# A transformer block in fp32: the first MLP product by a seven-product scheme over two batches, activations kept transposed, attention in pairs of heads

## Chip, cores, metric

The kernel runs on one core of a Trainium2 chip. The metric is the device time of one launch in microseconds (us), as the median over runs. A profile is one execution of the program, recorded by the hardware profiler.

## The reference

Inputs are q, k, v of 4 batches, 12 heads, 448 positions and 64 columns a head, and two MLPs of width 768 with 3072 hidden units. Everything is fp32.

```python
# attention, per batch and head
q_n, k_n = rmsnorm(q, g_q), rmsnorm(k, g_k)
attn = softmax(q_n @ k_n.T / sqrt(64))
x = attn @ v                                  # heads side by side: 4 x 448 x 768
# first MLP, behind a layer norm
xn = (x - mean(x)) / sqrt(var(x) + 1e-6) * g_ln
x = x + maximum(xn @ w_ch1, 0) @ w_ch2        # 768 -> 3072 -> 768
# second MLP, behind a mixing of positions of rank 32
u = x + (x.T @ U @ V).T
out = u + maximum(u @ w_ch1b, 0) @ w_ch2b
```

## The kernel before

**Number format.** A large product is made of three matmuls in the single-pass format float32r: an operand is split into a high part (a copy by ScalarE, written as float32r) and a low part (a subtraction by VectorE), and high x high, high x low and low x high are added up in PSUM. Transposes and the product of the softmax weights with v are plain fp32.

**Attention** (function `attention`, L105 to L557) runs over 48 heads, a loop of steps with software pipelining: each engine has its own `step`, in which it works on up to four heads at different stages. The order on TensorE is written out by hand in `step` (L337): scores of head n-1 (L296, L297), transposes of the exponentials of head n-2 (L308), products with v of heads n-3 and n-2 (L322), transposes of K of head n (L333). For the scores the high and low part of q lie one above the other, 128 rows, and K is held twice (L274), so that a tile of scores needs two matmuls of 448 columns, against the high and the low part of K. ScalarE computes the exponentials (L372), VectorE the maxima (L444), copies half of the transposed weights out of PSUM (L463) and makes low parts (L469, L476). POOL squares q and K (L249), takes the root of the means with a power (L253, L267) and normalises K (L271). SP issues all loads. The result x stays in SBUF in natural layout, positions on partitions.

**MLPs** (function `mlps`, L560 to L956) are 8 stages, one for each MLP and batch. A stage loops over 24 tiles j of 128 hidden units: `hidden` (L721) makes one hidden tile in 18 matmuls of 448 columns (6 tiles of the input x 3 terms, L733), ScalarE and VectorE apply the maximum with zero and split it (L817, L932), and `output` (L737) adds its part to the six PSUM banks of the output in 18 more (L750). The hidden tile of j+1 comes ahead of the output of j, so that TensorE need not wait. Weights of one j (two transfers of 384 KB, L98 and L99) are loaded once for each batch and split anew each time: two high parts of 768 columns on ScalarE (L781, L782), two low parts on VectorE (L844, L845). They wait for ring slots (`w_free`). Between output tiles TensorE does side work (`side`, L684): it transposes the finished output of the stage before back to natural layout (L680), where VectorE adds it to x (L891), mixes positions (L698, L706) and, at the end of a stage, transposes the next batch's input (L669), which ScalarE and VectorE split (L786, L851, L854). The first batch's input is built after the attention (L658). At the end the last output is transposed back (L680), added (L891) and stored (L832).

## Time and profile before

| | |
|---|---|
| runs, device time | 1797.34, 1797.57, 1797.84 us; median 1797.57 |
| profiled execution, span from its first to its last instruction | 1794.6 us |
| TensorE busy | 1766.4 us, 98% |
| VectorE, ScalarE, POOL busy | 913.4, 706.3, 202.1 us |
| read from and written to memory | 173.5 MB, 5.5 MB |
| first matmul of an MLP product | 344.8 us |
| granted TensorE clock, mean | 0.998 |

The page of the profiled execution gives its span alone. The median of the runs is 2.97 us above it: what lies around the span. A matmul's recorded duration holds its way through the pipeline, so the distance between starts tells what one costs. In a row, L750 is line 750 of the kernel, PE is TensorE, DVE VectorE, ACT ScalarE.

### The profile page before, as it was taken

The page shows a single profiled execution, that of the slowest core. Times are in us where ns is not written, and L with a number is a line of the kernel's source. Part 1 is how long each engine was busy: PE and PEld are TensorE (multiplying, and loading weights), DVE is VectorE, ACT ScalarE, POOL GpSimd, SP SyncE. Part 2 cuts the span into 40 slices and gives each one's busy share as a digit, 9 for nine tenths or more (in the row PEclk, how much of TensorE's full clock was granted, in tenths as well). Part 3 has the DMA queues.
Part 4 walks back from the last instruction along what each step waited for, and adds up shares of the span by engine and source line. Part 5 has one row for each costly group of instructions (what it writes and reads, how often), then busy time and mean ns, then how long its engine had stood idle before and what let it go on. Part 6 is the DMA issues. An engine that isn't in the chain of part 4 may idle for free.

```text
span 1794.6 us, 29017 instructions
## 1 busy us (share of the span) xinstructions
PE 1766.4 (98%) x10272; PEld 1655.9 (92%) x10272; DVE 913.4 (51%) x1595; ACT 706.3 (39%) x1268; POOL 202.1 (11%) x201
## 2 busy tenths in 40 slices
PE   6999999999999999999999999999999999999998
PEld 5999999899999999999999999999999999999997
DVE  7999999743344444444444444444433433343332
ACT  5777777522333323332333233323222322232221
POOL 6666666000000000000000000000000000000000
PEclk9999999999999999999999999999999999999999
DMA  2222224233333233333333333332433333333320
GB/s 73 69 69 72 68 71 139 87 106 116 113 106 103 93 111 101 106 106 106 105 108 100 102 100 106 106 106 89 138 121 106 97 131 121 106 99 128 121 88 31
DMA packets 205744, 180.41 MB, mean 101 GB/s; under 512 B 12497, under 2 KB 179281, under 8 KB 205649
## 3 DMA queue, kind: packets, MB, share of 16 engines
q1 hardware_dynamic: 203280, 173.51, 30.3%
q10 hardware_dynamic: 2368, 5.51, 0.8%
q8 instruction: 75, 1.23, 0.3%
q14 instruction: 21, 0.16, 0.0%
HBM read 173.48 MB, written 5.51 MB: 100 GB/s over the span
## 4 chain that ended last, share of the span: by engine, by line
PE 80%; DVE 0%; issue 0%; ACT 0%
PE h_ps L733 39%; PE y_ps L750 38%; PE h_ps L680 1%; PE h_ps L669 1%; PE h_ps L698 1%; PE h_ps L706 0%; PE y_ps L658 0%; DVE in_nat L891 0%; ACT in_hi L786 0%; DVE in_lo L854 0%; DVE in_lo L851 0%; DVE y_t L927 0%
## 5 line engine op out<-in xcount | busy, mean ns | idle before, releaser
L844 DVE TENSOR_TENSOR w_lo<-w_raw,w_hi 128x768 fp32r<-128x768 f32 x190 | 182.0, 958 | 674.0 <-ACT w_hi L782 674.0
L750 PE MATMUL y_ps<-h_hi,w_hi 128*128 128x448 f32 x1152 | 424.4, 368 | 0.0
L733 PE MATMUL h_ps<-in_hi,w_hi 128*128 128x448 f32 x1152 | 415.9, 361 | 3.1 <-DVE in_lo L851 1.1
L733 PE MATMUL h_ps<-in_hi,w_lo 128*128 128x448 f32 x1152 | 417.9, 363 | 0.0
L750 PE MATMUL y_ps<-h_hi,w_lo 128*128 128x448 f32 x1152 | 417.8, 363 | 0.0
L750 PE MATMUL y_ps<-h_lo,w_hi 128*128 128x448 f32 x1152 | 417.7, 363 | 0.0
L733 PE MATMUL h_ps<-in_lo,w_hi 128*128 128x448 f32 x1152 | 417.4, 362 | 0.0
L781 ACT ACTIVATE w_hi<-w_raw 128x768 fp32r<-128x768 f32 x189 | 159.7, 845 | 538.1 <-PE y_ps L750 538.1
L817 ACT ACTIVATE h_hi<-h_ps 128x448 fp32r<-128x448 f32 x192 | 104.7, 545 | 380.1 <-PE h_ps L733 338.5
L733 PEld LDWEIGHTS h_ps<-in_hi,w_hi 128*128 128x128 f32 x1152 | 215.6, 187 | 19.1 <-DVE in_lo L851 1.5
L733 PEld LDWEIGHTS h_ps<-in_lo,w_hi 128*128 128x128 f32 x1152 | 216.2, 188 | 15.8
L750 PEld LDWEIGHTS y_ps<-h_lo,w_hi 128*128 128x128 f32 x1152 | 216.7, 188 | 14.0
L750 PEld LDWEIGHTS y_ps<-h_hi,w_hi 128*128 128x128 f32 x1152 | 215.9, 187 | 13.5
L750 PEld LDWEIGHTS y_ps<-h_hi,w_lo 128*128 128x128 f32 x1152 | 216.1, 188 | 13.0
L733 PEld LDWEIGHTS h_ps<-in_hi,w_lo 128*128 128x128 f32 x1152 | 216.1, 188 | 12.4
L845 DVE TENSOR_TENSOR w_lo<-w_raw,w_hi 128x768 fp32r<-128x768 f32 x190 | 180.7, 951 | 0.0
L322 PEld LDWEIGHTS av_ps<-v_nat,e_t 112*112 112x112 f32 x1536 | 172.7, 178 | 5.2
L322 PE MATMUL av_ps<-v_nat,e_t 112*112 112x64 f32 x1536 | 174.2, 257 | 0.0
L782 ACT ACTIVATE w_hi<-w_raw 128x768 fp32r<-128x768 f32 x189 | 156.4, 827 | 0.0
L932 DVE SCALAR_TENSOR_TENSOR h_lo<-h_ps,h_hi 128x448 fp32r<-128x448 f32 x192 | 118.9, 619 | 71.6 <-ACT h_hi L817 70.9
L372 ACT ACTIVATE e_nat<-scores,nbias,rs_all 112x448 f32<-112x448 f32 x192 | 138.0, 721 | 40.3 <-DVE nbias L452 40.2
L444 DVE TENSOR_REDUCE nmax<-scores 112x1 f32<-112x448 f32 x192 | 113.2, 615 | 4.3 <-PE scores L297 1.6
(90 smaller groups left out, 1407.3 us busy)
## 6 DMA issues: line engine op xcount, KB each, us to landing
w_raw<-in_moe_w_ch SPq DMA_DIRECT2D x384, 384.0 KB, 3.8
qk_raw<-in_q SPq DMA_DIRECT2D x48, 112.0 KB, 2.0
qk_raw<-in_k SPq DMA_DIRECT2D x48, 112.0 KB, 2.1
qt_raw<-in_q_t SPq DMA_DIRECT2D x48, 112.0 KB, 2.5
v_nat<-in_v SPq DMA_DIRECT2D x48, 112.0 KB, 2.0
out<-o_nat ACTq DMA_DIRECT2D x12, 336.0 KB, 5.0
out<-in_nat ACTq DMA_DIRECT2D x4, 336.0 KB, 3.1
u_sb<-in_moe_U SPq DMA_DIRECT2D x4, 56.0 KB, 2.5
```

The lines of the kernel that those rows point to most:

```text
L322: last = nc.tensor.matmul(av_ps[:TP, m * D:(m + 1) * D], e_t[:, m, c, :], v_nat[:, slot, c, :], start=(c == 0), stop=(c == NI - 1))
L372: nc.scalar.activation(e_nat[:, i, :], scores[i][:TP, :S], ACT.Exp, bias=nbias[:, i:i + 1], scale=rs_all[:, ds(g, 1), i:i + 1].rearrange(" ...
L444: nc.vector.reduce_max(nmax[:, i:i + 1], scores[i][:TP, :S], axis=AX, negate=True).then_inc(rawmax_done, 1)
L669: last = nc.tensor.transpose(h_ps[c % 2][:, i * TP:(i + 1) * TP], in_nat[:, i, c * P:(c + 1) * P], ident[:TP, :TP])
L733: last = nc.tensor.matmul(h_ps[j % 2][:, :S], w[:, j % NW, c, :], x[:, c, :], start=(c == 0 and t == 0), stop=(c == DC - 1 and t == 2))
L750: last = nc.tensor.matmul(y_ps[c][:, :S], w[:, j % NW, c * P:(c + 1) * P], x[:, j % 2, :], start=(j == 0 and t == 0), stop=(j == FC - 1 an ...
L781: nc.scalar.activation(w1_hi[:, r], w1_raw[:, r], ACT.Copy)
L782: nc.scalar.activation(w2_hi[:, r], w2_raw[:, r], ACT.Copy).then_inc(w_hi_done, 1)
L817: nc.scalar.activation(h_hi[:, j % 2, :], h_ps[j % 2][:, :S], ACT.Relu).then_inc(hhi_done, 1)
L844: nc.vector.tensor_tensor(w1_lo[:, r], w1_raw[:, r], w1_hi[:, r].bitcast(F32), ALU.subtract)
L845: nc.vector.tensor_tensor(w2_lo[:, r], w2_raw[:, r], w2_hi[:, r].bitcast(F32), ALU.subtract).then_inc(w_lo_done, 1)
L932: nc.vector.scalar_tensor_tensor(h_lo[:, j % 2, :], h_ps[j % 2][:, :S], 0.0, h_hi[:, j % 2, :].bitcast(F32), ALU.max, ALU.subtract).then_i ...
```

## The change

The kernel is rewritten. The parts on which the steps of the prediction rest:

- **Products.** A stage now holds one MLP and two batches: 4 stages. The two batches, the two halves of the 768 inputs and two hidden tiles make a 2 x 2 x 2 block product, done by Strassen's scheme in the form with 7 products (named P1 to P7) of sums of blocks instead of 8. Each is 3 input tiles x 3 terms, 9 matmuls of 448 columns. There are 12 groups a stage. POOL makes 4 sums of weight blocks a group (`weight_sum`, 384 columns), ScalarE and VectorE split 7. P2, P3 and P4 accumulate onto the banks of P1, P5 and P7. VectorE combines the rest with 5 adds (`combine`), ScalarE copies P1 out (`keep_p1`), and 4 hidden tiles get their high and low parts. The second product stays plain: after each 2 groups 12 products of 12 matmuls, of which each second closes two banks that VectorE adds to the residual (`gather`). Splits are done 3 to 4 products ahead of use, in a ring of 8. A weight transfer is now one of 786 KB for 7 or for 6 products (a run), requested two products before the end of the run before the last, into one of two buffers.
- **Inputs of a stage.** They are sums of blocks too: for each of 3 tiles 4 sums on POOL (`make_sums`), 7 high parts on ScalarE and 7 low parts on VectorE (448 columns), made during the last second product of the stage before, and for the first stage in steps 66 to 97 of the attention (of 96 steps and 6 of draining). Normalised x and x go through memory (`xnrm`, `xres`), 229 KB a tile.
- **Transposed activations.** x is transposed once after the attention and once more normalised (4 transposes a pair each, for the last 6 pairs normalised during the first stage). Outputs are never transposed back; the host lays the result out. The residual of a stage (`acc`, 2.75 MB) is loaded from memory from the 8th product of a stage on (`load_acc`). The mixing is done in stages 1 and 2 in 12 items that last 22 products each: 8 transposes, 8 matmuls of 256 columns, 2 of 448.
- **Attention in pairs of heads.** 24 pairs x 4 steps. For the scores the two heads lie in rows 0 to 63 and 64 to 127; a step has 3 terms x 2 heads of 64 rows, alternating between the heads, into two banks. One maximum on VectorE reads both banks (896 columns), the root on POOL has 16 columns, K of both heads is transposed together (4 transposes a pair). The low part of q is made by POOL. TensorE runs the scores of step n, then values of step n-2 and transposes of step n-1 for either head.
- **Idle TensorE fed.** Matmuls whose result is not used (`warm`): 36 before the first transposes, 5 after them, 13 in steps 1 to 3. The first products of the first stage are placed between the last steps of the attention (`seq`).

The diff, cut to these parts:

```diff
+P1, P7, P6, P5, P2, P3, P4 = range(7)
+ORDER = (P1, P7, P6, P5, P2, P3, P4)
+ONTO = {P2: P1, P3: P5, P4: P7}
+LAST_IN_BANK = (P6, P2, P3, P4)
+
+OUTS = ((0, 0), (1, 0), (2, 0), (0, 1), (1, 1), (2, 1), (3, 0), (3, 1), (4, 0), (4, 1), (5, 0), (5, 1))
...
+    prods = []
+    for s in range(STAGES):
+        for j in range(NJ):
+            for g in (2 * j, 2 * j + 1):
+                prods += [("G", s, g, k) for k in ORDER]
+            prods += [("M", s, j, n) for n in range(len(OUTS))]
...
+    make_at = {}
+    for c, first in enumerate((66, 77, 88)):
+        for off in range(-2, 8):
+            make_at.setdefault(("step", first + off + off // 3), []).append((0, c, off))
+    for s in range(1, STAGES):
+        first = number["M", s - 1, NJ - 1, 0]
+        for c in range(HC):
+            for off in range(-2, 8):
+                make_at.setdefault(("prod", first + (0, 3, 5)[c] + off), []).append((s, c, off))
...
+    seq = []
+    for n in range(STEPS):
+        seq.append(("step", n))
+        if 58 <= n < 63:
+            seq.append(("pre", n - 63))
+        if n >= N:
+            seq.append(("prod", n - N))
+    seq += [("prod", q) for q in range(STEPS - N, Q)]
...
+                def load_weights(r):
+                    if r >= len(runs):
                         return
+                    if r >= 2:
+                        sp.wait_ge(wlo_done, runs[r - 2][-1] + 1)
+                    kind, s, n, k = prods[runs[r][0]]
+                    src = w1[s // 2, n].rearrange("p a c -> p (a c)") if kind == "G" else w2[s // 2, n, k // 6]
+                    sp.dma_start(w_raw[r % 2][:].rearrange("p a c -> p (a c)"), src).then_inc(w_in[r % 2], 16)
...
+                def load_acc(s):
...
+                    for b in range(2):
+                        sp.dma_start(acc[:, b], xres[2 * (s % 2) + b].rearrange("c p s -> p c s")).then_inc(acc_in, 16)
...
+                def root(t):
+                    pool.wait_ge(ms_done, t + 1)
...
+                    nc.gpsimd.tensor_tensor(rs[:, t % 2].rearrange("p a h i -> p (a h i)"), qk_ms[:],
+                                            m_half[:TP], ALU.pow).then_inc(rs_done, 1)
...
+                def norm_k(t):
+                    pool.wait_ge(rs_done, t + 1)
+                    nc.gpsimd.tensor_tensor(kn.rearrange("p i (h d) -> p h i d", h=2), qk[:, t % 2, 1],
+                                            rs[:, t % 2, 1].unsqueeze(3).to_broadcast([TP, 2, NI, D]),
+                                            ALU.mult).then_inc(kn_done, 1)
...
+                def weight_sum(r, k):
+                    weights_in(pool, r)
...
+                    if k == P5:
+                        if old is not None:
+                            pool.wait_ge(wlo_done, product_of(old, P5) + 1)
+                        out, in0, in1, op = w_s1[:], a21, a22, ALU.add
+                    if k == P7:
+                        pool.wait_ge(sum_done, sum_no[r, P5] + 1)
+                        out, in0, in1, op = a21, a11, a21, ALU.subtract
+                    if k == P6:
+                        if old is not None:
+                            pool.wait_ge(wlo_done, product_of(old, P3) + 1)
+                        pool.wait_ge(sum_done, sum_no[r, P5] + 1)
+                        out, in0, in1, op = w_s2[:], w_s1[:], a11, ALU.subtract
+                    if k == P3:
+                        pool.wait_ge(sum_done, sum_no[r, P6] + 1)
+                        pool.wait_ge(wlo_done, product_of(r, P6) + 1)
+                        out, in0, in1, op = w_s2[:], a12, w_s2[:], ALU.subtract
+                    nc.gpsimd.tensor_tensor(out, in0, in1, op).then_inc(sum_done, 1)
...
+                def score(n):
+                    t, i = divmod(n, NI)
                     if i == 0:
-                        pe.wait_ge(klo_done, g + 1)
-                        pe.wait_ge(qlo_done, g + 1)
-                    wait(pe, exp_done, NI * g + i - NI + 1)
-                    lhs = q_st[:, slot, i * TP:(i + 1) * TP]
-                    nc.tensor.matmul(scores[i][:TP, :S], lhs, k_hi[:, slot, :], start=True, stop=False)
-                    nc.tensor.matmul(scores[i][:TP, :S], lhs, k_lo[:, slot, :], start=False,
-                                     stop=True).then_inc(scores_done, 1)
-
-                def turn_exp(pair, n, m):
-
-                    if not real(pair, n):
-                        return
-                    g = head(pair, n)
-                    pe.wait_ge(exp_done, NI * g + m + 1)
-                    wait(pe, et_odd if m % 2 else et_even, 2 * g + m // 2)
+                        emptied(pe, "k", t)
+                        pe.wait_ge(qlo_done, t + 1)
+                    wait(pe, exp_done, 2 * (n - 1))
+                    for a, b in ((q_hi, k_hi), (q_hi, k_lo), (q_lo, k_hi)):
+                        for h in range(2):
+                            rows = slice(h * D, (h + 1) * D)
+                            last = nc.tensor.matmul(mm_ps[:TP, 2 * (n % 2) + h, :S], a[rows, t % 2, i * TP:(i + 1) * TP],
+                                                    b[rows, t % 2], start=a is q_hi and b is k_hi, stop=a is q_lo)
+                    last.then_inc(s_done, 1)
+
...
+                def value(n, h):
...
+                    emptied(pe, "e", n, h)
+                    cols = slice((h * NI + i) * D, (h * NI + i + 1) * D)
                     for c in range(NI):
+                        last = nc.tensor.matmul(mm_ps[:TP, 4 + t % 2, cols], e_t[h][:, c * TP:(c + 1) * TP],
+                                                v[:, t % 2, h, c], start=c == 0, stop=c == NI - 1)
+                    last.then_inc(val_done, 1)
...
+                def product(q):
+                    kind, s, n, k = prods[q]
...
+                            read_out(pe, *old)
+                    w = w_hi[:, q % RING], w_lo[:, q % RING]
+                    if kind == "G":
+                        for c in range(HC):
+                            if n == 0:
+                                pe.wait_ge(inlo_done[c], made(s, k))
+                            for p, (a, x) in enumerate(((0, in_hi), (0, in_lo), (1, in_hi))):
+                                last = nc.tensor.matmul(bank(q), w[a][:, c * P:(c + 1) * P], x[:, k, c],
+                                                        start=k not in ONTO and c == 0 and p == 0,
+                                                        stop=c == HC - 1 and p == 2, skip_group_check=k in ONTO)
+                    else:
+                        d, half = OUTS[k]
+                        if d == 0:
+                            pe.wait_ge(hlo_done, 4 * (s * NG + 2 * n + half + 1))
+                        for b in range(2):
+                            for c in range(2):
+                                for p, (a, x) in enumerate(((0, h_hi), (0, h_lo), (1, h_hi))):
+                                    last = nc.tensor.matmul(bank(q, b), w[a][:, c * P:(c + 1) * P], x[:, half, 2 * c + b],
+                                                            start=half == 0 and c == 0 and p == 0,
+                                                            stop=half == 1 and c == 1 and p == 2)
+                    last.then_inc(prod_done, 1)
...
+                def mixing(item, off):
+                    i, part = divmod(off - 7, 3)
...
+                        pe.wait_ge(xslo_done, NI * item + i + 1)
+                        for x in (xs_hi, xs_lo):
+                            last = nc.tensor.matmul(sc_ps[1][:, :2 * P], u_st[:, i].rearrange("p n r -> p (n r)"), x[:],
+                                                    start=i == 0 and x is xs_hi, stop=i == NI - 1 and x is xs_lo)
+                        last.then_inc(z_done, 1)
...
+                            wait(pe, mu_done, 2 * item)
+                        wait(pe, xslo_done, NI * item + i)
+                        for e in range(2):
+                            last = nc.tensor.transpose(sc_ps[0][:TP, e * P:(e + 1) * P], xa[:, e, i * TP:(i + 1) * TP],
...
+                            pe.wait_ge(v_ok, 1)
+                        pe.wait_ge(mixlo_done, item + 1)
+                        for e in range(2):
+                            nc.tensor.matmul(sc_ps[e][:, :S], mix[:, e * P:(e + 1) * P], v_mx[:], start=True,
+                                             stop=True).then_inc(mo_done, 1)
...
+                def warm(times):
+                    for _ in range(times):
+                        nc.tensor.matmul(mm_ps[:, 5, :P], ident[:], ident[:], start=True, stop=True)
...
+                warm(36)
+                turn_k(0)
+                warm(5)
+                for what, n in seq:
+                    if what == "step":
+                        if n < N:
+                            score(n)
+                        if 1 <= n <= 3:
+                            warm((7, 3, 3)[n - 1])
+                        for h in range(2):
+                            if 0 <= n - 2 < N:
+                                value(n - 2, h)
+                            if 0 <= n - 1 < N:
+                                turn_e(n - 1, h)
+                        if n % NI == 2 and n // NI + 1 < NP_:
+                            turn_k(n // NI + 1)
+                        if xt_pair(n) is not None:
+                            turn_x("x", xt_pair(n))
+                        if xn_pair(n) is not None:
+                            turn_x("n", xn_pair(n))
+                    if what == "prod":
+                        if ln3_pair(n - 2) is not None:
+                            turn_x("n", ln3_pair(n - 2))
+                        if (at := mix_of(n)):
+                            mixing(*at)
+                        product(n)
...
+                def maximum(n):
+                    t, i = divmod(n, NI)
...
+                    nc.vector.reduce_max(nmax[:, n % 2], mm_ps[:TP, 2 * (n % 2):2 * (n % 2) + 2, :S], axis=AX,
+                                         negate=True).then_inc(max_done, 1)
...
+                    nc.vector.tensor_tensor(nbias[:, n % 2], nmax[:, n % 2], rs[:, t % 2, 0, :, i],
+                                            ALU.mult).then_inc(nb_done, 1)
...
+                def weight_low(q):
+                    dve.wait_ge(whi_done, q + 1)
+                    w = width(q)
+                    nc.vector.tensor_tensor(w_lo[:, q % RING, :w], weights(q), w_hi[:, q % RING, :w].bitcast(F32),
+                                            ALU.subtract).then_inc(wlo_done, 1)
...
+                def combine(q):
+                    g, k = g_no(q), prods[q][3]
+                    if k not in COMB or k == P7:
+                        return
+                    dve.wait_ge(prod_done, q + 1)
+                    if k == P6:
+                        dve.wait_ge(p1_done, g + 1)
+                        nc.vector.tensor_tensor(t_u2, bank(q), t_u2, ALU.add).then_inc(comb_done, 1)
+                        dve.wait_ge(comb_done, 5 * g + 1)
+                        wait(dve, hlo_done, 4 * g)
+                        nc.vector.tensor_tensor(t_c22, bank(number[prods[q][:3] + (P7,)]), t_u2, ALU.add
+                                                ).then_inc(comb_done, 1)
+                        return
+                    if k == P5:
+                        dve.wait_ge(comb_done, 5 * g + 2)
+                        nc.vector.tensor_tensor(t_c22, bank(q), t_c22, ALU.add).then_inc(comb_done, 1)
+                    if k == P3:
+                        nc.vector.tensor_tensor(t_c12, bank(q), t_u2, ALU.add).then_inc(comb_done, 1)
+                    if k == P4:
+                        nc.vector.tensor_tensor(t_c21, bank(q), t_u2, ALU.add).then_inc(comb_done, 1)
...
+                def gather(q):
+                    _, s, j, k = prods[q]
+                    d, half = OUTS[k]
+                    if not half:
+                        return
+                    dve.wait_ge(prod_done, q + 1)
+                    if s and j == 0 and d == 0:
+                        dve.wait_ge(acc_in, 32 * s)
+                    for b in range(2):
+                        nc.vector.tensor_tensor(acc[:, b, d], bank(q, b), acc[:, b, d], ALU.add).then_inc(ev_done, 1)
```

## Rows read from the trace of the kernel before

**Rows 1.** The page, busy time of each engine in us, its share, instructions.

```profile
PE 1766.4 (98%) x10272; PEld 1655.9 (92%) x10272; DVE 913.4 (51%) x1595; ACT 706.3 (39%) x1268; POOL 202.1 (11%) x201
```

**Rows 2.** Two stretches: busy us and instructions by engine, granted clock, DMA share, GB/s.

```profile
100.00:200.00 100.00, 100.00 (x915) 95.99 (x913) 94.75 (x229) 78.05 (x184) 63.50 (x63) 1.00 0.25 70
...
500.00:1000.00 500.00, 498.85 (x2568) 466.60 (x2567) 223.52 (x329) 166.12 (x255) 2.01 (x2) 1.00 0.32 103
```

**Rows 3.** The page, lines of the chain that ended last, share of the span.

```profile
PE h_ps L733 39%; PE y_ps L750 38%; PE h_ps L680 1%; PE h_ps L669 1%; PE h_ps L698 1%; PE h_ps L706 0%; PE y_ps L658 0%; DVE in_nat L891 0%; ACT in_hi L786 0%; DVE in_lo L854 0%; DVE in_lo L851 0%; DVE y_t L927 0%
```

**Rows 4.** Groups of TensorE instructions: shapes, count, busy us, mean ns, idle before.

```profile
L733 PE MATMUL h_ps<-in_lo,w_hi 128*128 128x448 f32 x1152 | 417.4, 362 | 0.0
...
L322 PE MATMUL av_ps<-v_nat,e_t 112*112 112x64 f32 x1536 | 174.2, 257 | 0.0
...
L308 PE MATMUL et_ps<-ident,e_nat 112*112 112x112 f32 x768 | 98.5, 261 | 0.4 <-ACT e_nat L372 0.4
```

**Rows 5.** Timeline of one head in attention, TensorE: start us, us.

```profile
199.72 0.44 PE L296 MATMUL scores<-k_hi,q_st 128*112 128x448 f32 x1
...
200.20 0.55 PE L308 MATMUL et_ps<-ident,e_nat 112*112 112x112 f32 x4
...
200.59 0.91 PE L322 MATMUL av_ps<-v_nat,e_t 112*112 112x64 f32 x8
...
201.34 0.56 PE L333 MATMUL kt_ps<-ident,kn 112*128 112x112 f32 x4
...
201.66 0.44 PE L296 MATMUL scores<-k_hi,q_st 128*112 128x448 f32 x1
...
201.94 0.36 PE L297 MATMUL scores<-k_lo,q_st 128*112 128x448 f32 x1
...
206.30 0.44 PE L296 MATMUL scores<-k_hi,q_st 128*112 128x448 f32 x1
```

**Rows 6.** Pieces of the chain in order of time: start us, us.

```profile
344.79 7.22 PE h_ps L733 x36
...
534.84 3.61 PE y_ps L750 x18
542.38 3.61 PE y_ps L750 x18
...
1777.60 7.22 PE y_ps L750 x36
```

**Rows 7.** Groups of VectorE and ScalarE instructions, columns as in Rows 4.

```profile
L372 ACT ACTIVATE e_nat<-scores,nbias,rs_all 112x448 f32<-112x448 f32 x192 | 138.0, 721 | 40.3 <-DVE nbias L452 40.2
L932 DVE SCALAR_TENSOR_TENSOR h_lo<-h_ps,h_hi 128x448 fp32r<-128x448 f32 x192 | 118.9, 619 | 71.6 <-ACT h_hi L817 70.9
L444 DVE TENSOR_REDUCE nmax<-scores 112x1 f32<-112x448 f32 x192 | 113.2, 615 | 4.3 <-PE scores L297 1.6
...
L900 DVE TENSOR_TENSOR xs_lo<-x_all,xs_hi 112x384 fp32r<-112x384 f32 x32 | 16.9, 549 | 0.0
```

**Rows 8.** POOL: two groups of instructions, columns as in Rows 4.

```profile
L249 POOL TENSOR_TENSOR qk_sq<-qk_raw 112x512 f32<-112x512 f32 x47 | 48.9, 1040 | 0.0
...
L649 POOL TENSOR_TENSOR rstd<-var_eps,m_half 112x4 f32<-112x4 f32 x3 | 3.0, 1007 | 468.1 <-DVE var_eps L868 468.1
```

**Rows 9.** Timeline of the start, POOL and VectorE, and TensorE's first score.

```profile
9.28 1.64 POOL L267 TENSOR_TENSOR rs_all<-qk_ms,m_half 112x8 f32<-112x8 f32 x1 [1.50 <-DVE qk_ms L488]
...
14.14 0.62 DVE L476 TENSOR_TENSOR q_st<-qt_raw,q_st 64x448 fp32r<-64x448 f32 x1
14.19 2.07 POOL L267 TENSOR_TENSOR rs_all<-qk_ms,m_half 112x8 f32<-112x8 f32 x1 [1.00 <-DVE qk_ms L488]
...
15.53 0.71 PE L296 MATMUL scores<-k_hi,q_st 128*112 128x448 f32 x1 [6.00 <-DVE k_lo L469]
```

**Rows 10.** Timeline of the end: the last adds on VectorE.

```profile
1789.74 1.02 DVE L891 TENSOR_TENSOR in_nat<-h_ps,x_all 112x384 f32<-112x384 f32 x2 [0.17 <-PE h_ps L680]
```

**Rows 11.** The page, DMA issues: out<-in, queue, count, KB each, us to landing.

```profile
w_raw<-in_moe_w_ch SPq DMA_DIRECT2D x384, 384.0 KB, 3.8
```


## Prediction before the result

> **What bounds the kernel now.** I read the page's busy line first, then stretches, then the chain, then single instructions. TensorE is busy for 98% of the span [rows 1]; attention and MLP stretches separately show it at 100% and 99.8%, with VectorE at 95% in attention but 45% in the MLPs, and the granted clock at 1.00 in both [rows 2], which is the upper of its two levels, 2.4 GHz. The chain of waits has 77% of the span in the two product lines L733 and L750 [rows 3]. Busy time is modelled, so I take the pace from starts. Eighteen matmuls of a product take 3.61 us and 36 take 7.22 us [rows 6], so one costs 0.200 us although its row says 362 ns [rows 4]. In attention one head lasts from 199.72 to 206.30, 6.58 us [rows 5]. Inside it nothing is missing: 4 transposes take 0.39 us (0.098 each), 8 value matmuls 0.75 (0.094 each), the 4 of K 0.32 (0.08 each) [rows 5]. The value line has 1536 matmuls for 48 heads [rows 4], so each of the 16 of a head is two instructions. 32 values are 3.0 us, 16 transposes 1.6, K 0.3, which leaves 1.7 for 8 scores, 0.21 each. TensorE bounds everything, and the time is a count of its instructions.
>
> By stage: first product matmul at 344.8 [rows 6]; then 6912 of them x 0.200 = 1382; the last 36 start at 1777.60 and end at 1784.8, so the MLP stretch of 1440 us holds 58 us of other work. One piece of it: two neighbouring blocks lie 7.54 us apart where 36 matmuls need 7.20 [rows 6], so three transposes cost 0.34. After 1784.8 come 9.8 us of tail, the last two adds starting at 1789.74 [rows 10].
>
> **The products.** One group is two hidden tiles for two batches. It cost 2 x 2 x 18 = 72 matmuls and costs 7 products x 9 = 63. 4 stages x 12 groups x 63 = 3024 against 3456. The second product stays at 4 x 6 x 12 x 12 = 3456. 6480 x 0.200 = 1296, 86 us less. This is the main gain.
>
> What must hide behind it. VectorE, per group: 5 combining adds and 4 low parts at 0.62 (448 columns, L932), 7 weight splits of 384 columns at 0.55 (L900) [rows 7]: 9.4 us of the 12.6 that TensorE needs. ScalarE has 12 copies; at 0.72, what an exponential of 448 columns costs [rows 7], they are 8.6, an upper bound. POOL: 4 sums of 384 columns; 512 columns take 1.04 [rows 8], so about 0.8 each, 3.3 in all. The tightest wait is P3, which accumulates onto P5's bank: P5 ends 1.8 us before P3 begins, and VectorE has a 0.55 split (done while P5 still runs) and the 0.62 add in between, so 1.0 us is left. All is covered: cost nothing. If that slack goes, each group pays the excess. The second product has 28.8 us per j for 12 splits of 256 columns (0.15 + 256 x 1.04 ns = 0.42, by the line through L900 and L444 [rows 7]) and 12 adds of 0.62: 12.5.
>
> **Other TensorE work in the MLPs.** Gone: the transposes back and those that build inputs. Added: 12 mixing items of 8 transposes (0.113 each with switching, from the 0.34), 8 matmuls of 256 columns (0.13; between 0.094 and 0.200), 2 of 448, 7 interruptions of 0.07: 2.8 us each, 34; 6 late transpositions, 3. Together 37, before 58.
>
> **Stalls at the seams.** Inputs of the next stage are made during the last second product: 21 VectorE subtractions of 0.62 = 13.0 beside its own 12.5, so 25.5 of 28.8. POOL adds 12 sums at 0.93 = 11. What both engines do to each other is in the trace. The root over 8 columns takes POOL 1.64 us at 9.28, and 2.07 us at 14.19, where VectorE began a two-operand subtraction at 14.14 [rows 9]: it lost 0.43 us to an instruction of 0.62. If all of it excluded each other a seam would need 36.7 us of 28.8, 7.9 late; if none, 0. I take 4 for each of 3 seams. The Trainium skill, SBUF — State Buffer, section Who interferes with whom, calls this an exclusive lock of the port that the two engines share; the trace agrees with those 0.43 us. The reload of the 2.75 MB residual starts 12.6 us into a stage and is wanted at about 35; 384 KB land in 3.8 us [rows 11], so even seven one after another take 27, and one behind the other on the queue about 13. Between 0 and 5 us a stage I take 2. Seams and reloads: 18.
>
> **Attention.** Per pair of heads, TensorE now: 64 values 6.0; 32 + 4 + 3 transposes (weights, x, normalised x in 18 of 24 pairs) x 0.098 = 3.8; K 0.3, since both heads share 128 columns; and 24 score matmuls of 64 rows. No row of the trace has two matmuls in the array at once. Bounds: two heads together, 12 x 0.21 + 4 x 0.08 for a fresh start = 2.8; one after another, 24 x 0.21 + 0.3 = 5.3. The nearest rows, matmuls of full height, come one after another, but those compete for the same rows of the array; these two use different halves and write different banks, so I take 2.8 and keep 5.3 as a rival. Pair: 12.9. VectorE per pair: 4 maxima of 896 columns (1.08, by the same line) with their bias 0.2, 4 copies 0.61, the sum of squares 1.4, the output 0.7, statistics 1.1, K 0.7, small 0.6: 12.0. It must follow TensorE step by step at 91%, so I add 0.3: 13.2 a pair, before 13.16.
>
> The start: load 5 us (448 KB in one transfer; 384 KB take 3.8 [rows 11]), squares 2.0, mean 1.4, root of 16 columns 2.9 (4 columns 1.0 and 8 columns 1.64, so 0.16 a column [rows 8, 9]), K 1.1, transposing and splitting it 1.8: first score at 14.2, before 15.53 [rows 9]. The second pair repeats squares, mean, root, K on POOL and VectorE, so its first score is at about 25.6. Then 23 x 13.2 = 304, to 329. The first stage's inputs (13 us VectorE over 8 pairs that have 9.6 free, and half of POOL's 11) add 9: 338. Step 96 costs 2.2, steps 97 to 101, which run between the first products, 2.5: 343, before 344.8. So attention is worth nothing by itself.
>
> **The tail:** the last two adds 1.3, a store of 229 KB about 3.5: 5, before 9.8.
>
> **Sum.** 343 + 1296 + 37 + 18 + 5 = 1699 us of span. The profile of before has 1794.6 and its runs a median of 1797.57, 3.0 more, which I carry over: **1702 us**, a gain of 5.3%.
>
> **Rivals.**
> Scores one after another (0.20). For it: no row shows overlap. Attention becomes TensorE-bound again, so the 0.3 a pair goes: 24 x (2.5 - 0.3) = 53, 1755 us. Switching between matmuls of 64 and of 128 rows, 192 times, is priced above by 0.08, what L296 at 201.66 pays over L297 [rows 5]. The Trainium skill, TensorEngine Tiling (Array Packing), section Tiling Modes, says that a change of mode drains the engine, which speaks against this change and gives no price. Its page TensorE: Matmul & The Clock Gate, Part 3, has tiles of different rows run side by side; nothing before shows either.
>
> VectorE and POOL in each other's way at full price (0.14). Seams 7.9 instead of 4, attention 5.6 more, and 0.5 us in each of 48 groups, where a sum of 0.8 and a split use up the 1.0 us before P3: 12 + 6 + 24 = 42, 1744 us. Against: POOL had 1.04 us for its squares in the mean over 47 [rows 8], beside a VectorE at 95%.
>
> Attention set by the hand-overs (0.11). A step is 3.3 us and VectorE's worst (maximum, output, statistics, copy) is 3.7. At 14.5 us a pair: 31 more, 1733 us. For it: VectorE was at 95% already [rows 2].
>
> Slower: weights come late (0.04). A run's 786 KB are requested about 7 us before POOL and ScalarE, both in order, want them; ScalarE's wait then holds the hidden tiles behind it, so from about 9 us on TensorE pays the excess in each of 96 runs. At 10 us the gain is gone; at 11 us it is 192 us, 1894 us. The acc, input and mixing transfers share the queue. Against: 384 KB land in 3.8 us [rows 11], so 786 KB in about 6, and the MLPs moved 103 GB/s at a DMA share of 0.32 [rows 2], while the new weights are 786 KB per 13.5 us, 58 GB/s.
>
> That the change doesn't shorten the product is excluded, since the matmuls are counted in the code.
>
> **Chances.** Forecast 0.50, the rivals 0.20, 0.14, 0.11, 0.04, 0.01 for no change. The forecast's own range is 1670 to 1730 (a pair of 12.5 to 13.8, stalls of 0 to 30). Taking in serial scores and the full price of the port, 1662 to 1772. A measurement tells 0.2%, 3.6 us, from no change. Faster 0.95, within 0.2% 0.01, slower 0.04.
>
> **What would show it.** Matmuls of a product 0.200 us apart, and 54.0 us for two groups with their second product; the second stage near 324 + 17 us long; scores of two heads starting within 0.1 us of each other, or 0.2 if the rival holds; first score near 14; first product near 340; POOL's sums longer than 0.8 where they meet VectorE's subtractions. Wrong if TensorE idles inside groups on VectorE's add of P5, or on weight splits behind a DMA, or if the granted clock falls.

## The result and the profile after

The changed kernel takes 1844.78 us (median of 1818.59, 1851.84, 1854.31 and 1837.71), the kernel before 1797.46 beside it: a ratio of 1.0173, 95% interval 1.0118 to 1.0228. The ratio leaves out the two executions over 1.5% above the fastest (1851.84 and 1854.31 us), as all ratios here do; the medians alone give 1.026. It is **slower by 1.7%**, where 1702 us, 5.3% faster, was forecast, with 0.04 on slower. The executions differ in the granted clock of TensorE, 0.941 to 0.962 over the whole span; before it was 0.998. The profiled one is the fastest, with a span of 1816.8 us.

The page of the changed kernel, busy line and granted clock in 40 slices, against [rows 1]:

```profile
PE 1772.3 (98%) x9972; PEld 1598.1 (88%) x9972; DVE 1121.1 (62%) x2088; ACT 683.0 (38%) x1588; POOL 495.3 (27%) x419
...
PEclk9999965588999999999999999999999999999999
```

TensorE is as busy as before. The second row holds the finding: the clock is low in slices 6 to 10, from 227 us on, which is attention up to its end at some 430 us. Stretches of the changed kernel (columns as in [rows 2]):

```profile
100.00:150.00 50.00, 49.65 (x458) 42.01 (x457) 39.83 (x85) 33.01 (x84) 31.94 (x23) 1.00 0.27 78
...
200.00:220.00 20.00, 16.75 (x134) 14.38 (x135) 14.33 (x29) 9.99 (x24) 10.84 (x10) 0.83 0.21 62
...
300.00:320.00 20.00, 20.00 (x103) 17.23 (x103) 11.43 (x21) 8.84 (x21) 9.42 (x6) 0.50 0.08 24
320.00:340.00 20.00, 20.00 (x103) 17.23 (x103) 11.01 (x24) 8.54 (x21) 3.67 (x3) 0.50 0.30 84
```

At 0.50 (1.2 of 2.4 GHz) TensorE is busy in all 20 us and does 103 instructions, where at 1.00 it does some 180. A reader of the busy share alone sees nothing wrong. The first matmul of a product is the first start of this line of the source (min, median, max ns, then first and last start):

```profile
L696 PE MATMUL mm_ps<-in_hi,w_hi x1008: 362/365/575, 431.6 to 1782.7; 128*128 128x448 f32 x168
```

431.6 us, forecast 343, so 89 of the 118 us that the span is over its forecast (1816.8 against 1699) arise in attention. Up to 180 us attention runs at a clock of 1.00, with two heads side by side and no wait above 0.1 us after the first steps. TensorE in one step:

```profile
100.16 0.46 PE L643 MATMUL mm_ps<-k_hi,q_hi 64*112 64x448 f32 x2
100.45 0.36 PE L643 MATMUL mm_ps<-k_lo,q_hi 64*112 64x448 f32 x2
100.65 0.37 PE L643 MATMUL mm_ps<-k_hi,q_lo 64*112 64x448 f32 x2
100.95 1.00 PE L663 MATMUL mm_ps<-v,e_t 112*112 112x64 f32 x8
101.78 0.55 PE L651 MATMUL sc_ps<-ident,e_nat 112*112 112x112 f32 x4
...
102.92 0.55 PE L651 MATMUL sc_ps<-ident,e_nat 112*112 112x112 f32 x4
103.39 0.46 PE L643 MATMUL mm_ps<-k_hi,q_hi 64*112 64x448 f32 x2
```

Six score matmuls take 0.79 us, the step 3.23. Then, around 200 us, all engines:

```profile
198.23 3.12 POOL L586 TENSOR_SCALAR x_nat<-x_nat,moments,rstd 112x128 f32<-112x128 f32 x4
...
201.46 0.84 DVE L994 BATCH_NORM_AGGREGATE moments<-stats 112x2 f32<-112x36 f32 x4 [4.45 <-POOL x_nat L586]
202.34 0.17 DVE L998 TENSOR_SCALAR var<-moments 112x4 f32<-112x4 f32 x1
202.41 0.62 DVE L962 COPY e_t<-sc_ps 112x448 f32<-112x448 f32 x1
...
203.18 0.97 PE L651 MATMUL sc_ps<-ident,e_nat 112*112 112x112 f32 x4 [3.35 <-DVE e_t L962]
```

VectorE's aggregate waits 4.45 us for POOL's normalisation, the copy that frees a scratch bank is queued behind it, TensorE idles 3.35 us, and its next transposes last 0.97 us instead of 0.55: half the clock. Thirty us later comes another chain:

```profile
232.31 0.99 POOL L579 TENSOR_TENSOR w_raw<-w_raw 128x384 f32<-128x384 f32 x1
232.32 1.00 DVE L957 TENSOR_TENSOR nbias<-nmax,rs 112x2 f32<-112x2 f32 x1
233.24 0.67 DVE L943 SCALAR_TENSOR_TENSOR k_lo<-sc_ps,g_qk,k_hi 128x448 fp32r<-128x448 f32 x1
...
234.06 0.57 PE L651 MATMUL sc_ps<-ident,e_nat 112*112 112x112 f32 x4 [1.98 <-DVE k_lo L943]
```

A product of two columns, 0.16 us elsewhere, takes 1.00 us and ends with POOL's weight sum. It is followed by k_lo, which frees the bank of the keys, and a turn of normalised x stands in that same step, so TensorE needs the bank earlier than in other steps.

### The profile page after: what moved, and what is told of

Same layout as the page of the kernel before. It is cut to its first block, busy times and chain, and to the rows that moved or that the text cites. A ratio compares the mean times of both kernels' runs of the same rounds, so it can differ in the third digit from the quotient of the medians.

```text
span 1816.8 us, 27033 instructions
## 1 busy us (share of the span) xinstructions
PE 1772.3 (98%) x9972; PEld 1598.1 (88%) x9972; DVE 1121.1 (62%) x2088; ACT 683.0 (38%) x1588; POOL 495.3 (27%) x419
## 4 chain that ended last, share of the span: by engine, by line
PE 87%; DVE 8%; POOL 2%; DMA 1%; issue 1%; ACT 1%; SPq 0%; DVEq 0%; ACTq 0%; POOLq 0%
PE mm_ps L706 35%; PE mm_ps L696 31%; PE mm_ps L663 9%; PE mm_ps L643 4%; PE sc_ps L651 4%; DVE in_lo L1012 3%; PE sc_ps L674 1%; POOL x_nat L586 1%; DVE acc L1052 1%; DVE w_lo L1003 1%; PE sc_ps L718 1%; POOL qk_sq L517 1%; PE mm_ps L743 1%; DMA xres<-xa 1%; DVE h_lo L1019 1%
## 5 line engine op out<-in xcount | busy, mean ns | idle before, releaser
L706 PE MATMUL mm_ps<-h_hi,w_hi 128*128 128x448 f32 x1152 | 424.0, 368 | 10.3 <-DVE w_lo L1003 9.7
L706 PE MATMUL mm_ps<-h_hi,w_lo 128*128 128x448 f32 x1152 | 421.6, 366 | 0.0
L706 PE MATMUL mm_ps<-h_lo,w_hi 128*128 128x448 f32 x1152 | 421.6, 366 | 0.0
L696 PE MATMUL mm_ps<-in_hi,w_hi 128*128 128x448 f32 x1008 | 372.1, 369 | 2.3 <-DVE w_lo L1003 1.2
L696 PE MATMUL mm_ps<-in_hi,w_lo 128*128 128x448 f32 x1008 | 368.5, 366 | 0.0
L696 PE MATMUL mm_ps<-in_lo,w_hi 128*128 128x448 f32 x1008 | 368.4, 365 | 0.0
L706 PEld LDWEIGHTS mm_ps<-h_hi,w_hi 128*128 128x128 f32 x1152 | 216.5, 188 | 29.8 <-DVE w_lo L1003 11.6
L706 PEld LDWEIGHTS mm_ps<-h_hi,w_lo 128*128 128x128 f32 x1152 | 216.7, 188 | 17.8
L706 PEld LDWEIGHTS mm_ps<-h_lo,w_hi 128*128 128x128 f32 x1152 | 216.8, 188 | 17.3
L1003 DVE TENSOR_TENSOR w_lo<-w_raw,w_hi 128x256 fp32r<-128x256 f32 (+1 forms) x480 | 231.0, 493 | 0.2
```

The source lines that it names most:

```text
L696: last = nc.tensor.matmul(bank(q), w[a][:, c * P:(c + 1) * P], x[:, k, c], start=k not in ONTO and c == 0 and p == 0, stop=c == HC - 1 and ...
L706: last = nc.tensor.matmul(bank(q, b), w[a][:, c * P:(c + 1) * P], x[:, half, 2 * c + b], start=half == 0 and c == 0 and p == 0, stop=half ...
L1003: nc.vector.tensor_tensor(w_lo[:, q % RING, :w], weights(q), w_hi[:, q % RING, :w].bitcast(F32), ALU.subtract).then_inc(wlo_done, 1)
```

## Theory and rivals

**Theory:** TensorE has no slack in attention (busy 99% of it), so a few waits of 1 to 3 us, made by POOL's normalisation, by VectorE operations held up beside POOL, and by a turn in the step of the keys, let the granted clock fall; the half clock, which then holds for long although TensorE is fully busy, costs far more than the waits. **Rival A:** the work that overlaps attention from about 180 us on is simply too much for POOL and VectorE. **Rival B:** single waits matter, but only one cause does (POOL's time, or the hold-up on nbias). **Rival C**, the one that the expectations of runs 1 and 2 call thin feed: attention in pairs of heads keeps TensorE so thinly fed that the clock falls whatever the waits do. The seams and the pace of the products are separate questions.

## Experiments

**1. The turns of batch 0 end earlier.** XN_AT, batch 0:

```diff
-(0, 4, 8, 12, 16, 20)
+(0, 4, 8, 12, 14, 16)
```

> Theory (stalls let the granted clock fall, and half the clock costs attention its time): the last normalised pair of the first batch is turned one step group earlier, so VectorE's aggregate at 201 us no longer waits 4.4 us for POOL and TensorE's 3.35 us gap at 199.6 goes. The clock stays 1.00 from 180 to about 230; whether it falls behind that depends on the next stall, at 231 to 234, where POOL is over-full. First product matmul between 370 and 425 us (changed kernel: 431.6), time 1760 to 1815. Rival (attention in pairs feeds the array too thinly, the clock falls whatever the stalls do): clock at or below 0.9 in 180 to 230, first product at 430, 1815 to 1855.

1856.64 us, clock 0.932 in the profiled execution (span 1869.0), first product at 479.2. The aggregate no longer stopped TensorE, but one of the moved turns fell into a step in which keys are turned:

```profile
184.32 0.96 PE L651 MATMUL sc_ps<-ident,e_nat 112*112 112x112 f32 x4 [1.76 <-DVE k_lo L943]
```

The clock fell there, 17 us earlier than in the changed kernel (184 instead of 201 us), and stayed at 0.50 until 276. So the place of a turn decides where the clock falls. What it costs these runs don't tell: the first product is 48 us later than in the changed kernel, but that compares the slower of two executions (1842.53 and 1870.74) with the fastest of four (1818.59 to 1854.31), and the ranges overlap. The forecast of 370 to 425 us for the first product missed, and clock and time came out as rival C had them; runs 3 and 7 decide that.

**2. The same, and x is normalised on ScalarE.**

```diff
-last = nc.gpsimd.tensor_scalar(x, x, moments[:, i, 0:1], rstd4[:, i:i + 1], ALU.subtract, ALU.mult)
+last = nc.scalar.activation(x, x, ACT.Identity, bias=nmr4[:, i:i + 1], scale=rstd4[:, i:i + 1])
```

> As the first, and the normalisation of x in the attention is done by ScalarE (about 0.3 us for each of 4) instead of POOL (0.8 each). POOL is relieved by 3.1 to 6.2 us a pair. Theory: no TensorE gap over 2 us in attention up to the making of the first stage's inputs; clock 1.00 up to about 290 us; first product at 345 to 375, time 1725 to 1765. Rival (thin feed): clock still falls to 0.5 for tens of us, first product over 400, time over 1800.

The diff is shortened: VectorE also negates the mean, and POOL multiplies it by the root.

1868.61 us (1835.92 to 1873.70), a miss again. ScalarE takes 488 ns a tile and not the 0.3 us expected, 1.95 us a pair, against POOL's 3.12. The same wait of 1.76 us on k_lo is at 184.63, the clock falls there, first product at 477.3. POOL's time on x had no part in this fall. The collision of turn and keys had, but not alone: in both runs nbias, just ahead of it, takes 0.78 us instead of 0.16 (at 182.8 and at 183.1).

**3. The wait at 203 is filled.** Thirteen matmuls on the identity before the late transposes:

```diff
+if n == 52 and h == 0:
+    warm(13)
```

> The changed kernel with 13 unused matmuls (26 instructions, about 3 us) placed where TensorE waits at 199.6 us; nothing is made faster. Theory: the wait is as long, but the granted clock stays 1.00 from 200 to 230 (changed kernel 0.50 at 204 to 208), and 2 to 4 us are won there. Rival (POOL's and VectorE's lateness, not the idle array, is what costs): no change in the clock in this stretch and none in time before 230 us.

1830.06 us, ratio 1.0185 (1.0164 to 1.0206). TensorE, and then two stretches:

```profile
199.76 3.12 PE L743 MATMUL mm_ps<-ident 128*128 128x128 f32 x26
203.28 0.57 PE L651 MATMUL sc_ps<-ident,e_nat 112*112 112x112 f32 x4 [0.41 <-DVE e_t L964]
```

```profile
204.00:212.00 8.00, 8.00 (x79) 7.01 (x77) 6.79 (x17) 5.63 (x15) 4.91 (x3) 1.00 0.24 68
...
227.00:240.00 13.00, 11.39 (x68) 9.76 (x67) 5.52 (x9) 6.27 (x16) 11.95 (x13) 0.67 0.30 90
```

The delay was the same, but with TensorE fed through it the clock stayed at 1.00 from 204 to 212, where it was 0.74 in the changed kernel. So it is the idling that lets it fall, against rival C. It fell later, after waits of 0.46 and 1.15 us on e_t and k_lo at 227 and 231; the first product came at 440.4. One wait filled bought no time that can be told (1827.63 and 1832.48 us lie within the four of the changed kernel), since the next took its place.

**4. No sums of input blocks after the first stage** (the kernel leaves out POOL's `make_sums` for stages 2 to 4).

> POOL's sums of input blocks at the three seams between stages are left out (the blocks go in unsummed, so the output is another); waits and counts stay. Theory (POOL and VectorE exclude each other on two-operand work in SBUF): the low parts of the inputs fall from 1.28 and 1.00 us to 0.62 at the seams, and TensorE's idle time of 2.4, 5.1 and 4 to 5 us there goes nearly to 0: the stretch from the first product to the end falls from 1385 us by 8 to 13. Rival (VectorE alone is too full at the seams, or the loads from memory are late): low parts as long as before or idle time stays within 3 us of 12.

From the first product to the end 1376.5 us (1828.2 less 451.7), against 1385.2 in the changed kernel: 8.7 us. VectorE's low parts, first of the changed kernel, then of this one:

```profile
L1012 DVE TENSOR_TENSOR in_lo<-make_a,in_hi 128x448 fp32r<-128x448 f32 x21 | 26.9, 1282 | 12.3 <-ACT in_hi L838 12.3
L1012 DVE TENSOR_TENSOR in_lo<-make_b,in_hi 128x448 fp32r<-128x448 f32 x21 | 21.1, 1004 | 0.0
```

```profile
L1015 DVE TENSOR_TENSOR in_lo<-make_a,in_hi 128x448 fp32r<-128x448 f32 x21 | 14.6, 695 | 10.3 <-ACT in_hi L841 10.3
L1015 DVE TENSOR_TENSOR in_lo<-make_b,in_hi 128x448 fp32r<-128x448 f32 x21 | 14.5, 690 | 0.0
```

Without POOL's sums they take 0.69 us instead of 1.28 and 1.00, and no wait above 0.5 us is left at the seams, where the changed kernel has 13 us of them. POOL and VectorE do stand in each other's way there. That 13 us became only 8.7 has mostly another reason. TensorE from 1500 to 1700 us, first of the changed kernel, then of this one:

```profile
1500.00:1700.00 200.00, 200.00 (x989) 1.00 0.20 66
```

```profile
1500.00:1700.00 200.00, 200.00 (x969) 1.00 0.20 70
```

From about 1450 us on this execution runs its products 0.2067 us apart and not 0.2027 (last section), which costs it some 7 us. It is one execution.

**5. All turns out of the steps of the keys**, and the last of batch 0 early enough for the aggregate:

```diff
-((0, 4, 8, 12, 16, 20), (0, 2, 4, 6, 8, 10), (0, 4, 8, 12, 14, 16))
+((0, 4, 8, 12, 13, 16), (0, 1, 4, 5, 8, 9), (0, 4, 8, 12, 13, 16))
-for u in (xn_pair(n + 1), xn_pair(n + 3)):
+for u in (xn_pair(n + 1), xn_pair(n + 2)):
```

> The turns of normalised x moved: batch 0 to the steps (0, 4, 8, 12, 13, 16) after its start, batch 1 to (0, 1, 4, 5, 8, 9), batch 2 to (0, 4, 8, 12, 13, 16), so that none stands in a step in which keys are turned, and POOL has normalised the last pair of batch 0 before VectorE's aggregate of batch 1 wants it. Nothing else changes; the same work is done. Theory (it is the two waits of 3.35 and 1.98 us at 203 and 234 us, with their kind further on, that let the granted clock fall, and the clock then costs the attention): no idle time of TensorE above 1 us between 100 and 250 us, the granted clock 1.00 in every stretch there, the first matmul of a product at 345 to 385 us instead of 431.6, a span of 1730 to 1770 us, faster than the kernel before. Rival (the work that overlaps attention from about 180 us on, block sums, low parts and weight sums on POOL and VectorE, is too much by itself, wherever the turns stand): other waits of 1 to 2 us appear at the same place, the clock falls there again, first product at 410 us or later, span above 1800 us.

1817.01 us, but from 1778.65 to 1832.14; the profile is of the slowest of the four. Here the numbers came out as the rival had them (first product at 437.2, over 1800 us), and still not for its reason: the wait of 3.35 us had gone and the clock held to 234; then the second turn came too soon after the first for POOL, which has two pairs in one piece:

```profile
234.56 1.01 PE L674 MATMUL sc_ps<-ident,x_nat 112*128 112x112 f32 x4 [2.95 <-POOL x_nat L586]
```

**6. Those places, and x on ScalarE**, a pair in the step before its turn.

> The same places of the turns as in the run before, and x is normalised on ScalarE, one pair in the step before its turn (488 ns a tile, four tiles a pair, 1.95 us) instead of on POOL (3.12 us a pair). Theory: POOL no longer delays the rs and K steps where two pairs are normalised together (6.25 us in one piece on POOL); ScalarE has 2.3 us of work in a step of 3.2 us, so a step with a normalisation is about 1 us too long for it and catches up in the next. If POOL was the limit, the first product comes 5 to 20 us earlier than in the run before; if ScalarE is late with the exponentials instead, TensorE shows waits on e_nat or nbias of about 1 us in those steps, the clock falls and the first product is later, 400 us or more.

1785.24 us, ratio 0.9936 (0.9917 to 0.9954): for the first time with its median under the kernel before. First product at 397.9, 39 us earlier than in run 5 and not 5 to 20, but run 5's fastest execution, 1778.65, is under both of these. The profile shows what is gained: no wait on x, and a clock of 1.00 up to 285. What ends it, on POOL, VectorE and TensorE:

```profile
283.59 1.89 POOL L520 TENSOR_TENSOR qk_sq<-qk 112x1024 f32<-112x1024 f32 x1
```

```profile
283.61 1.89 DVE L969 TENSOR_TENSOR nbias<-nmax,rs 112x2 f32<-112x2 f32 x1
285.42 0.67 DVE L955 SCALAR_TENSOR_TENSOR k_lo<-sc_ps,g_qk,k_hi 128x448 fp32r<-128x448 f32 x1
```

```profile
286.24 0.97 PE L653 MATMUL sc_ps<-ident,e_nat 112*112 112x112 f32 x4 [1.92 <-DVE k_lo L955]
```

The product of two columns starts 0.02 us after POOL's squares and lasts exactly as long as they do.

**7. nbias with one operand in SBUF.** Per head, rs as a scalar (shortened: without the semaphore updates):

```diff
-nc.vector.tensor_tensor(nbias[:, n % 2], nmax[:, n % 2], rs[:, t % 2, 0, :, i], ALU.mult)
+for h in range(2):
+    nc.vector.tensor_scalar(nbias[:, n % 2, h:h + 1], nmax[:, n % 2, h:h + 1],
+                            rs[:, t % 2, 0, h, i:i + 1], None, ALU.mult)
```

> The kernel of the run before (turns moved, x normalised on ScalarE), and nbias is made by two VectorE tensor_scalar of one column with rs as the scalar, in place of one tensor_tensor that reads nmax and rs from SBUF. In the run before nbias, 0.16 us by itself, took 1.89 us at 283.61, exactly until POOL's squares (283.59 to 285.48) ended; 0.86 at 264.47 and 0.75 at 268.94, until POOL's sums ended; k_lo came late behind it, TensorE waited 1.92 us and the granted clock fell to 0.50. Theory (a VectorE operation with two operands in SBUF waits until POOL's running instruction ends, one with a single operand doesn't): nbias takes under 0.2 us each time whatever POOL does; no wait of 1.9 us at 286, first product 15 to 50 us earlier than 422 us, so at 370 to 407 us; span 1730 to 1768 us against 1783.1. Rival (POOL slows every VectorE operation, or the wait is just of load): nbias still takes up to 1.9 us, or other operations take its place, clock falls at 286, span within 5 us of 1783.

The expectation's 422 us for the run before is a slip: its profile has the first product at 397.9.

1759.78 us, ratio **0.9793** (0.9766 to 0.9820), clock 0.997 or 0.998 in all four executions. nbias in the changed kernel, and here (min, median, max ns):

```profile
L957 DVE TENSOR_TENSOR nbias<-nmax,rs x96: 161/163/1881, 16.6 to 427.7; 112x2 f32<-112x2 f32 x96
```

```profile
L970 DVE TENSOR_SCALAR nbias<-nmax,rs x192: 203/210/217, 16.6 to 362.2; 112x1 f32<-112x1 f32 x192
```

Of 192 not one takes over 0.22 us, whatever POOL does. The same stretch as above, TensorE alone (time, busy time, instructions, clock, DMA share, GB/s):

```profile
320.00:340.00 20.00, 19.02 (x177) 1.00 0.32 104
```

With the clock kept it does 177 instructions where the changed kernel did 103. First product at 367.3. Rival C falls: the pairs are the same, and attention keeps its clock. So does rival A, except for one part: all the overlapping work is still there, but x is normalised on ScalarE and not on POOL. Run 11 puts it back.

**8. Low parts of the inputs last in VectorE's step** (shortened: without conditions and loops).

```diff
-aggregate(t // PB - 1)
-make_low(s, c, off)
 copy_e(n - 1)
+aggregate(t // PB - 1)
+make_low(s, c, off)
```

> As the run before, and on VectorE a step's copy of the transposed exponentials goes ahead of the aggregate and of the low part of the inputs (in_lo, two operands in SBUF, so it still waits for POOL: 1.80 us at 270.20), which come last in the step. Theory: the bank of PSUM is freed up to 1.8 us earlier in the steps with input blocks, so that the waits of TensorE on e_t, k_lo and st_x of 0.4 to 1.2 us in the last 120 us of attention get shorter; clock 1.00 up to 343 to 360 us, first product there, span 1728 to 1750 us. Rival: the delay only moves to the maximum of the next step and from there to nbias and e_nat; waits of 1 us remain, the clock falls, no gain over the run before.

1779.89 us, slower than run 7, a miss. ScalarE and TensorE:

```profile
296.92 0.58 ACT L840 ACTIVATE in_hi<-make 128x448 fp32r<-128x448 f32 x1 [3.97 <-DMA make<-xnrm]
```

```profile
298.07 1.08 PE L665 MATMUL mm_ps<-v,e_t 112*112 112x64 f32 x8 [2.59 <-ACT e_t L799]
```

The reload of that block:

```profile
290.11 1.75 SPq L415 DMA_DIRECT2D make<-xnrm  x4
```

In run 7 it is issued at 288.54. The low part of the inputs just before it starts at 289.39 here and at 287.82 there, so the buffer came free 1.6 us later. ScalarE, with its copy of e_t behind the block's high part, waited 3.97 us for the load instead of 2.86; TensorE waited 2.59 us instead of 0.86, and the clock fell at 298.

**9. The changed kernel with run 7's nbias alone.**

> The changed kernel itself with nothing but nbias made by two tensor_scalar. Theory that each wait above 1 us counts for itself: the wait of 3.35 us at 203 (VectorE's aggregate behind POOL's normalisation) stays, the clock falls there as before; of the waits on k_lo at 234, 280, 372, 389 and 409 those go that stood behind a long nbias (the 1.98 us at 234 among them); first product at 390 to 425 us instead of 431.6, span 1775 to 1810 us. Rival (the nbias wait is the whole cause): clock 1.00 from 100 to 340 us and a span below 1760 us.

1812.40 us, 1782.12 to 1852.68. The wait at 203 is 3.23 us and the clock falls there; the waits on k_lo shrink to 0.5 to 0.65, with the turns where they were. First product at 424.0. Rival B in its form "nbias alone" falls: no execution comes near 1760 us. The half clock after that one wait lasts 109 us here, from 203 to 312; after the wait of 3.35 us in the changed kernel it lasted 7. So a wait has no fixed price.

**10. Mixing first on VectorE.** Its part of a product goes ahead of weight splits, hidden tiles and blocks:

```diff
+if what == "prod" and (at := mix_of(n)):
+    mixing(*at)
 for q in low_at.get(n, ()):
     weight_low(q)
```

> The kernel with moved turns, x normalised on ScalarE and nbias by a scalar, and on VectorE the mixing's work of a product (xs_lo and the rest) goes ahead of the weight splits, hidden tiles and input blocks of that product instead of behind them. Theory: xs_lo was ready to run about 2 to 3 us earlier (xs_hi ended at 892.0, xs_lo started at 895.03 behind an h_lo that took 1.49 us beside POOL's weight sum), so the waits of TensorE on xs_lo, 0.3 to 1.3 us each and some 12 us over the two stages, go; seams are unchanged at about 3.1 + 0.9 + 0.6 + 0.5 us. Span 1746 to 1753 us against 1760.4. Rival: weight splits come later in those products and TensorE waits for w_lo instead, span within 3 us of 1760.

1748.44 us, ratio **0.9737** (0.9720 to 0.9753), the fastest kernel here, 2.6% under the one before. The wait on xs_lo, in the last column the idle time before it, of the changed kernel and here:

```profile
L718 PE MATMUL sc_ps<-xs_hi,u_st 112*128 112x256 f32 x48 | 15.8, 329 | 10.2 <-DVE xs_lo L1058 10.2
```

```profile
L720 PE MATMUL sc_ps<-xs_hi,u_st 112*128 112x256 f32 x48 | 14.2, 296 | 0.1
```

10.2 us of waiting became 0.1. The two profiled spans differ by more, 18.6 us; some 6 of that is the slower pace of run 7's last 300 us (see the last section).

**11. Run 7 with x still on POOL.**

> Moved turns and nbias by a scalar, x normalised on POOL as in the changed kernel (no mixing change). It tells what normalising on ScalarE is needed for. Theory: with two pairs normalised in one piece of 6.25 us on POOL, the second turn waits for it as before (2.95 us at 234.56), the clock falls there whatever nbias does, and rises again sooner than with long nbias: first product 385 to 420 us, span 1775 to 1810 us, uneven from run to run. Rival (the lock on nbias was all): no stretch below 1.00, first product near 370 us, span near 1760 us.

1784.67 us, 1761.70 to 1804.05; three of the eight executions keep a clock of 0.995 or 0.996 and take 1761.70 to 1768.19. In the profiled one TensorE waits 2.88 us on POOL's x at 234.80, the clock falls to 0.91 over 220 to 260 and to 0.62 over 300 to 340, this time behind a wait of 1.51 us on ScalarE's e_t; the first product is at 386.3. Rival B falls in its other form too, though not in each execution: the three look as it says. With x on POOL the clock is sometimes kept, so the overlapping work isn't by itself too much (rival A); with x on ScalarE it is kept in all four of run 7, 25 us less in the median. Runs 6 and 7 show the same of nbias. That the moved turns are needed beside these two is not shown: no run has x on ScalarE and nbias by a scalar with the old turns.

**12. Scores over all 128 rows** (each is then the sum of both heads').

```diff
-rows = slice(h * D, (h + 1) * D)
+rows = slice(0, 2 * D)
```

> The run before the last (mixing first) with the score matmuls of both heads over all 128 rows instead of 64 rows each, so that no matmul of the program uses half of the array's rows; each score is then the sum of both heads' scores, so this leaves out the separation of the heads, with the same number of instructions. It prices two things. First, two heads side by side: six score matmuls took 0.79 us, with about 0.08 more on each side; six of full height should take 6 x 0.2 = 1.2 us, a step 3.4 to 3.6 us instead of 3.23, a pair 0.5 to 1.5 us longer, first product at 380 to 400 us instead of 367; if the two do not overlap in fact, the step stays at 3.23 or gets shorter. Second, the pace of the products: 0.2027 us in the changed kernel and all runs of it (0.2067 in parts), 0.2000 in the kernel before, at the same granted clock. If the half-height matmuls in attention leave the array in a state that costs this, it returns to 0.2000 here and the stretch of the products is 17 us shorter (1357 instead of 1375); if they have nothing to do with it, it stays at 0.2027.

1768.78 us, against 1748.44 for run 10. One step:

```profile
104.12 0.63 PE L645 MATMUL mm_ps<-k_hi,q_hi 128*112 128x448 f32 x2
104.59 0.57 PE L645 MATMUL mm_ps<-k_lo,q_hi 128*112 128x448 f32 x2
104.99 0.56 PE L645 MATMUL mm_ps<-k_hi,q_lo 128*112 128x448 f32 x2
105.39 0.91 PE L665 MATMUL mm_ps<-v,e_t 112*112 112x64 f32 x8
...
107.27 0.55 PE L653 MATMUL sc_ps<-ident,e_nat 112*112 112x112 f32 x4
107.58 0.64 PE L645 MATMUL mm_ps<-k_hi,q_hi 128*112 128x448 f32 x2
```

Six scores take 1.27 us instead of 0.79, the value matmuls behind them 0.75 instead of 0.83, the transposes before them 0.32 (107.27 to 107.58) instead of 0.47, the step 3.46 instead of 3.23. First product 391.0 against 367.0. Two heads side by side are worth 24 us here, after paying for the change of height; part of it is a wait of 0.36 us on k_lo in nearly every pair, which run 10 doesn't have. The pace of the products stayed at 0.2027 (0.2067 from about 1440 us on).

## Why the prediction was wrong

**What held.** First score at 14.53 (14.2 forecast); scores of two heads together (the rival of 0.20, one after another, is refuted by the 0.79 us and by run 12); POOL's root 2.92 (2.9), the maximum of 896 columns 1.09 (1.08), K 1.04 (1.1); weights never late; no group stopped on VectorE's add of P5; the tail 4.5 us (last matmul 1812.27, span 1816.8; 5 forecast). The count of the products, the main gain, is real.

**The step that failed first: "Attention", the pair of 13.2 us, taken for all 24 pairs.** It failed in two ways.

*The change between matmuls of 64 and of 128 rows was priced at 0.08 us a step, and costs 0.24 more.* I wrote 2.8 us of scores for a pair, with 4 x 0.08 for a fresh start, and took that for the change's whole price. Measured at clock 1.00: scores 4 x 0.79 = 3.2, the first value matmuls 0.83 instead of 0.75, and the transposes before the scores 0.47 (102.92 to 103.39) instead of 0.39. The Trainium skill, TensorEngine Tiling (Array Packing), section Tiling Modes, says that a change of mode drains the engine; run 12 agrees: at full height the 0.08 after the scores is gone, and the transposes before them take 0.32. The 0.08 that I counted is something else, for at full height the start of the scores pays it still (two of them take 0.47, 104.12 to 104.59, where the next two take 0.40). A step is 3.23 us where my terms make 2.99 (0.71 + 1.50 + 0.78), so 23 us over 96 steps.

Run 7, at full clock until its first product, has it at 367.3, 24 us past my 343. That this is so near to 23 is partly luck. The 0.3 us a pair added for VectorE, 7 us, was not needed, since TensorE sets the pace; on the other side turns cost more than counted (in the changed kernel a pair with turns of K and x takes 14.0 us, with one of normalised x 14.6), and waits of 0.3 to 1.2 us come in from 230 us on. The rival "set by the hand-overs" had this size (14.5 a pair) with the wrong cause.

*The clock, the other 64 us of the profiled execution (431.6 less 367.3).* The text named "if the granted clock falls" among what would prove it wrong and gave it no chance and no price. I had no term for normalising x on POOL, 3.12 us a pair in 18 pairs, and didn't ask what waits behind it: VectorE's aggregate, the copy of e_t behind that, and TensorE. Nor did I price turns in the step of the keys. Each such wait cost 1 to 3 us itself; the half clock after them lasted some 130 us in all (the granted clock from 200 to 430 us is 0.71 in the mean), which loses 65 us of work. Not every such wait brings it: one of 1.16 us at 372.7 in the changed kernel left the clock at 1.00, one of 1.15 at 409.4 did not. A rival at these places, "TensorE idles 2 to 3 us and runs at 1.2 GHz until 430", would have had the right sign: it could have been built from the fact that attention has no slack. The other three executions lost still more, at clocks of 0.941 to 0.952.

**"VectorE and POOL in each other's way."** The mechanism was right and its worst place was missed. I priced it at seams and groups by the length of operations. It was dearest on an operation of 0.16 us that nobody would price: nbias, held for up to 1.88. The Trainium skill, SBUF — State Buffer, section Who interferes with whom, says that a VectorE instruction with two inputs in SBUF contends with a POOL instruction that reads SBUF, and that one with at most one such input, outside its two-port modes, doesn't; runs 6 and 7 agree, 1.89 us with two, never over 0.22 with one and a scalar.

**"Seams and reloads: 18."** The waits above 0.5 us at the three seams sum to about 13, and run 4, without POOL's sums, has none: against 12 forecast for what the two engines do to each other, that held in size and in cause. For the 6 of the reload no wait shows. But the waits on xs_lo, 10.2 us, stood in no term: I had costed the mixing on TensorE (37) and not its queue on VectorE.

**"6480 x 0.200 = 1296."** The count is right, the pace isn't: in long stretches of the changed kernel it is 0.2027, which makes 1314, 18 us more, at a granted clock of 1.00. With the 10 us of mixing that comes to the MLP stretch, 1385 instead of 1356, though the seams took 5 us less than forecast and as much elsewhere is not accounted for.

Together: 24 (switches, and what offsets in attention) + 64 (clock and waits in attention) + 18 (pace) + 10 (xs_lo) = 116 of the 118 us. The clock and the mixing were found by experiment, and so was the change of height inside the first term; the pace is measured and not explained.

**What is needed to have the gain:** turns placed away from the keys, x on ScalarE, nbias by a scalar and mixing first together give 1748.4 us (the part of the turns is not shown by itself). What is left against 1702 is mostly the 24 us in attention and 18 of pace.

## What to carry to other kernels

Where TensorE is busy all the time, look for the queues behind which a copy that frees its bank can stand, and price a wait there with the half clock that may follow, not with its own length; a busy share of 100% can hide this, so read the granted clock beside the count of instructions. On VectorE, give small operations beside a busy POOL a single operand in SBUF and the other as a scalar, and put what TensorE waits for first in the step. Count a change between matmuls of half and of full height at both borders of the stretch, behind it and ahead of it.

## What was not expected of the hardware

- Once at half clock, TensorE stayed there for long while it was busy all the time: from 300 to 340 us in the changed kernel at 0.50 with no idle time in the record, and it returned near 355 without a change in the work that I can see. What ends such a stretch stays open.
- The time of an execution then varies: 1782 to 1853 us over eight of run 9, 1762 to 1804 over eight of run 11, but 1756 to 1765 over four of run 7, which keeps its clock.
- Products have three paces at a granted clock of 1.00: 0.2000 us in the kernel before, everywhere; 0.2027 in all versions of the changed one; 0.2067 in parts, as in run 7 from 1420 us to the end, after the waits of a seam, and in run 4 from about 1450. Run 12 excludes the matmuls of half height as the cause. It stays open, and is worth 18 us; two versions that differ by less than 7 us can't be compared by their spans alone.
